# Attention and two feed-forward layers on one core: six tiles of 256 to 512 tokens in place of five of 384 to 512

## The reference, cut to what matters

```python
batch, n_heads, seq, head_dim = (4, 8, 576, 64)          # attention
n_tokens, d_model, d_ff = (2304, 512, 2048)              # first layer; the second has d_ff 1536

scores = 1/sqrt(64) * q @ k.T
scores = where(scores >= max(scores) - tau, scores, -1e9)
attn   = exp(scores - max) / (sum + 1e-9)
x      = (attn @ v), heads side by side                  # 2304 x 512

h  = x @ w_in;  x = (h * tanh(softplus(h))) @ w_out      # first layer (mish)
g  = x @ w_gate; out = (silu(g) * (x @ w_val)) @ w_out2  # second layer
```

## Time and profile before

| what | value |
|---|---|
| median of 3 runs | 1177.75 us |
| lowest run | 1173.86 us |
| the profiled execution | 1177.69 us, span 1175.9 us |
| busy PE / DVE / ACT / POOL | 96% / 51% / 49% / 51% of the span |
| moved by DMA | 231.85 MB, 197 GB/s over the span |
| mean granted clock | 0.984 |

### The profile page before, as it was taken

How to read it: one execution, slowest core, us unless ns; L and a number is a source line. 1 busy time by engine, 2 the same in 40 slices (tenths; PEclk the granted TensorE clock), 3 DMA queues, 4 the chain that set the end, 5 groups by cost and what they waited for, 6 DMA issues and landing times.

```text
span 1175.9 us, 17588 instructions
## 1 busy us (share of the span) xinstructions
PE 1128.5 (96%) x6096; PEld 1020.5 (87%) x6096; DVE 597.6 (51%) x1187; ACT 571.3 (49%) x1062; POOL 596.0 (51%) x777
## 2 busy tenths in 40 slices
PE   4667999999999999999999999999999999999998
PEld 4557999999999999998888888888888888999998
DVE  7883289886128877720287676200865552000220
ACT  6664778785456666613565455124544431330220
POOL 7663888987466666734554466324534432230220
PEclk9886999999999999999999999999999999999999
DMA  7311867766887676776554467656544445777673
GB/s 224 107 52 57 286 210 233 236 222 220 282 270 242 197 237 215 241 261 202 193 173 157 157 214 235 204 198 196 174 149 157 136 155 186 220 216 219 217 217 124
DMA packets 89512, 231.85 MB, mean 197 GB/s; under 512 B 10064, under 2 KB 27984, under 8 KB 89424
## 3 DMA queue, kind: packets, MB, share of 16 engines
q1 hardware_dynamic: 89280, 230.73, 60.7%
q10 hardware_dynamic: 144, 0.00, 0.0%
HBM read 190.32 MB, written 40.37 MB: 196 GB/s over the span
## 4 chain that ended last, share of the span: by engine, by line
PE 90%; POOL 4%; DVE 3%; issue 1%; ACT 1%; DMA 0%; SPq 0%; ACTq 0%; DVEq 0%
PE ps_m L564 23%; PE ps_m L566 23%; PE ps_m L565 23%; PE ps_x L617 7%; PE ps_s L588 3%; PE ps_s L589 3%; PE ps_x L629 3%; PE ps_x L628 3%; POOL p_t L941 1%; PE ps_m L617 1%; POOL k_lo L919 1%; DVE p_t L820 1%; PE ps_x L630 1%; DVE q_sp L807 1%; DVE nmax L813 1%
## 5 line engine op out<-in xcount | busy, mean ns | idle before, releaser
L564 PE MATMUL ps_m<-x_hi,w_sp 128*128 128x512 f32 (+2 forms) x800 | 301.9, 377 | 3.5 <-POOL x_lo L947 3.4
L566 PE MATMUL ps_m<-x_hi,w_sp 128*128 128x512 f32 (+2 forms) x800 | 296.5, 371 | 0.0
L565 PE MATMUL ps_m<-x_lo,w_sp 128*128 128x512 f32 (+2 forms) x800 | 296.1, 370 | 0.0
L564 PE MATMUL ps_m<-g_hi,w_sp 128*128 128x448 f32 (+2 forms) x560 | 211.5, 378 | 0.0
L565 PE MATMUL ps_m<-g_lo,w_sp 128*128 128x448 f32 (+2 forms) x560 | 207.1, 370 | 0.0
L566 PE MATMUL ps_m<-g_hi,w_sp 128*128 128x448 f32 (+2 forms) x560 | 207.1, 370 | 0.0
L820 DVE SCALAR_TENSOR_TENSOR p_t<-ps_s,thr,p_t 128x576 f32<-128x576 f32 x144 | 116.0, 816 | 119.8 <-ACT p_t L723 109.0
L564 PEld LDWEIGHTS ps_m<-x_hi,w_sp 128*128 128x128 f32 x800 | 150.8, 189 | 20.0 <-issue 4.0
L566 PEld LDWEIGHTS ps_m<-x_hi,w_sp 128*128 128x128 f32 x800 | 150.8, 188 | 18.1
L565 PEld LDWEIGHTS ps_m<-x_lo,w_sp 128*128 128x128 f32 x800 | 151.0, 189 | 15.3
L958 POOL TENSOR_TENSOR g_lo<-g_raw,g_hi 128x448 fp32r<-128x448 f32 (+2 forms) x80 | 96.2, 1204 | 97.9 <-ACT g_hi L749 97.5
(11 more groups left out here) (69 smaller groups left out, 1764.7 us busy)
## 6 DMA issues: line engine op xcount, KB each, us to landing
w_sp<-scratch SPq DMA_DIRECT2D x238, 512.0 KB, 3.8
scratch<-w_sp SPq DMA_DIRECT2D x68, 512.0 KB, 4.1
w_raw<-weights SPq DMA_DIRECT2D x102, 256.0 KB, 4.0
k_raw<-kt SPq DMA_DIRECT2D x64, 288.0 KB, 3.2
v_raw<-v SPq DMA_DIRECT2D x64, 160.0 KB, 3.2
q_raw<-qt SPq DMA_DIRECT2D x16, 192.0 KB, 3.4
out_t<-o_sb SPq DMA_DIRECT2D x8, 256.0 KB, 3.8
out_t<-o_sb SPq DMA_DIRECT2D x8, 224.0 KB, 3.5
```

What stands on the lines that cost most here:

```text
L564: nc.tensor.matmul(ps, w_h, x_h, start=first, stop=False)
L565: nc.tensor.matmul(ps, w_h, x_l, start=False, stop=False)
L566: return nc.tensor.matmul(ps, w_l, x_h, start=False, stop=last)
```

## The change

One line. The tiles keep their sum of 2304 and everything else follows from it. The pieces are then, by tile, 256 | 320 | 384 | 192, 320 | 256, 256 | 320, eight as before; the last tile (320) runs without attention beside it, as the last (448) did, and there are six passes over the weights where there were five, the sixth with reloads only.

```diff
-TILES = (384, 448, 512, 512, 448)
+TILES = (256, 320, 384, 512, 512, 320)
```

## The result

The kernel with six tiles takes 1180.09 us (median of 20 runs, 1176.58 to 1185.0), the one before 1175.6 us (median of 20 beside them): ratio 1.0037 with a 95% interval of [1.0025, 1.005]. It is 0.4% slower where 0.7% less was forecast. The time lies in the stated range of 1157 to 1194; the sign is the wrong one. The profiled execution has a span of 1179.0 us, 11 more than the sum of the prediction.

A forecast was written before the change was run, and what follows sets the result against it. Bound by a lead paced by VectorE and tile 0's attention chains, then TensorE's work at its own spacing. Span 1175.9 - 26 + 11.9 + 4 + 1 + 1 = 1167.8 us; forecast 1170 us, range 1157 to 1194.

The forecast's parts named there:

- term 4: DMA in the first two and last tiles: weight loads, stores and reloads near a possible 354 GB/s ceiling cost +1 us (0 to +5).
- Term 1: Lead before tile 0's first matmul: VectorE's work shrinks with fewer chunks and turns, -26 us (-16 to -31), lead of 78.
- Term 2: TensorE behind the lead: extra pass at 0.119 and 0.146 us a matmul, +4.2, and attention moved there, +7.7; together +11.9 us.
- Term 3: Tile 0: next attention squeezed beside narrower matmuls; VectorE fits barely, +4 us (0 to +10); ScalarE and GpSimd +1 (0 to +4).
- Rival 3: First two tiles starve as four raw weight slots come round too slowly; tile 0 at 160 us, total 1193; chance 0.15.
- Rival 4: Newly planned order leaves tile 1's attention late, TensorE stands still at the seam, +10 us: 1176; inside the forecast's shared 0.5.
- Rival 1: Lead no longer VectorE's but paced by k_low, v_low, loads and score banks; shrinks by only 16 us: 1180; chance 0.15.

The follow-up runs named there:

- a_lag5: Six-tile kernel with the planner allowing 5.0 us instead of 3.0 from a raw weight's load to its split, same instructions and bytes: ratio 0.9949 to the kernel before.
- a_thin: Six-tile kernel with stores and reloads of split weights cut to 256 columns of the high half, order unchanged: ratio 0.9979 to the kernel before.
- b_thin: Kernel before, with stores and reloads of split weights cut to 256 columns of the high half: ratio 1.0005 to the kernel before.
- b_lag5: Kernel before, with the planner allowing 5.0 us from a raw weight's load to its split: ratio 1.0018 to the unedited one.
- a_max: Six-tile kernel with the row maximum taken over 32 columns of each half of a score row, transfers unchanged: ratio 1.0013 to the kernel before.
- five_320: Kernel before with five tiles of 320, 448, 512, 512, 512: ratio 1.0165 to the kernel before.
- five_320b: Kernel before with five tiles of 320, 512, 512, 512, 448: ratio 1.0244 to the kernel before.
- a_raw6: Six-tile kernel with six raw weight slots in place of four: ratio 1.0042 to the kernel before.
- a_third: Six-tile kernel with the storing of split weights spread over three tiles in place of two: ratio 1.0255 to the kernel before.
- a_thin_norm: a_thin with the norm scaling only 64 of 576 columns besides: ratio 0.9935 to the kernel before.
- a_thin_max: a_thin with the row maximum over 32 columns of each half of a score row besides: ratio 0.9945 to the kernel before.

## Why the prediction was wrong

**The step that failed is term 4**, "I take +1 (0 to +5)", and the view behind it: "Were 354 a ceiling". It priced the transfers as a rate, bytes over GB/s, and nowhere asked when a load lands against where its consumer stands in ScalarE's order. 354 GB/s was no ceiling: tile 1's first 38 us, forecast at 374, moved 328 at a share of 0.91, and 10 us among them 380 at a share of 1.01,

```profile
227.00:265.10 38.10, 34.72 (x234) 33.80 (x233) 8.01 (x14) 21.11 (x46) 25.23 (x29) 1.00 0.91 328
...
250.00:260.00 10.00, 9.28 (x62) 8.85 (x62) 1.39 (x2) 6.03 (x15) 5.96 (x7) 1.00 1.01 380
```

and in a_lag5 the 10 us from 220 on moved 400. The median landing of a raw weight went from 4.0 to 4.5 us over the kernel, the longest stayed at 7.0, and the plan was drawn for 3.0. Before, the wider units left slack for that, 7.1 us from issue to split in tile 0; at 1.43 us a unit they leave 5.1. That the waits went by the order at the same bytes (a_lag5, -8.9 us) and by the bytes in the same order (a_thin, -10.3 us) is shown, by the ratios with -10.3 and -6.8; so is that the wider tiles don't have them (b_thin, b_lag5). How the cost splits into pauses and the clock that fell after one (some 1.7 us in tile 0) was not isolated. With this term at +10, the sum is 1177, beside 1179.0.

**Term 1 was right**: lead 78.0, -26.3 for -26. That VectorE bears on it is borne out by a_max, which shortens it by 4.9. That the forecast holds to a third of a microsecond is luck: b_lag5's lead is 6.3 us shorter than before's with more work on VectorE. The mechanism "goes with the tokens" is too simple all the same: at 320 tokens it is 99 to 101 us (five_320, five_320b).

**Term 2 was right in size**: 0.120 and 0.146 us a matmul in the feed-forward, so the pass costs what the value matmuls said; the whole is +13.7 for +11.9. The 2 us are within what the medians leave open: the scores (0.133), transposes (0.109) and value matmuls behind the lead add 8 us by them, for +7.7. The estimates from the Trainium skill (TensorE: Matmul & The Clock Gate, Wait — 56ns, not 53.3ns?), 0.109 and 0.136, are not what these matmuls do: they keep the 12 to 13 ns beyond their columns.

**Term 3 had the right size and the wrong place.** Tile 0 at 143 us with some waits came out with a_lag5 (143.4) and a_thin (143.2). But the waits that are left are not from VectorE's or GpSimd's load: the short maximum and the short norm take nothing off them that one profile shows. In tile 1, which had no term but a share of term 4's +1, 3 to 5 us are over its spacing in a_thin and a_lag5. One of them stands at its start; ScalarE, then TensorE, kernel after:

```profile
231.52 0.74 ACT L723 ACTIVATE p_t<-ps_s,nmax 128x576 f32<-128x576 f32 x1 [0.64 <-DVE nmax L813]
232.28 1.28 ACT L745 ACT_TABLE_LOAD   x1
233.58 0.77 ACT L745 ACTIVATE g_raw<-ps_m 128x320 f32<-128x320 f32 x2
...
234.16 0.39 PE L564 MATMUL ps_m<-x_hi,w_sp 128*128 128x320 f32 x1 [1.71 <-ACT g_raw L745]
```

The last exp of tile 0's stretch ends at 232.26, the table load takes 1.28 us, and the first `mish` comes only then; with units of 1.75 us and two banks for their results TensorE has run out. I read it as a cost of short units that the prediction had no term for; no run isolates it.

**The rivals.** None came as written. Rival 3 had the sign and the tiles, but its mechanism (slots that come round too slowly) is contradicted by a_raw6, and its own sign, "where tile 0 lasts longer than some 145 us", would have decided for it (149.0). Rival 4 is what a_third did. Rival 1 has the measured time, 1180, by another way: a lead 10 us longer than it is, so the match is chance. The rivals that were slower than the kernel before stood on the lead (1180) or on a collapse of 29 us in the first two tiles (1193), and none on a wait of 10 there, which is most of what turned -8 into +3.

**Open**: the 10 us over the spacing that tile 0 keeps even in a_lag5 (4.9 before), of which its start, 5.3 us at a granted clock of 0.50, is some 2.7 (before 4.3 us, some 2.2), and what the 4 us of a_thin_norm and a_thin_max under a_thin consist of. With a_lag5's order the span is 1170.1 for a forecast sum of 1167.8.

## What to carry to other kernels

Where a transfer's consumer stands in an in-order queue with other work behind it, price the landing time against the place in that queue, and not the bytes against a bandwidth: look for the engine's waits for DMAs, and for who stands behind them, even if that engine is half idle. When units get shorter, every fixed allowance of a static schedule (a landing, a table load, a semaphore) has to be looked at again; here one number, 3.0 to 5.0, turned 0.4% slower into 0.5% faster. And before a first tile is narrowed, count its turns and chunks: the lead falls in their steps and not with the tokens.

## What the runs showed of the hardware that I had not expected

The landing of a load depends on its company: 256 KB took 3.2 us in the median with thin stores and reloads beside it (shares of 0.61 and 0.46 in tiles 0 and 1), 4.0 before, 4.5 after (0.80 and 0.88). The longest took 7.0 us in both kernels. A matmul of 256 columns in the feed-forward kept its 0.120 us in a tile whose share of the transfers was 0.80. A share of 1.00 is no fixed rate: 354 GB/s in the busiest 10 us before, 380 after at 1.01. And a late split costs a second time: behind a pause of 1.85 us the granted clock stood at 0.50 for 3.4 us.
